# Moving two conversions of the input weights on ScalarE, and the row products ahead of the diagonal values on GpSimd, in the first loop of a fused attention and expert kernel

## The reference, cut to what matters

```python
for t in range(S):                                     # attention, B, H, S, D = 4, 8, 768, 48
    cur = np.einsum('bhd,bhe->bhde', u[None] * kt, vt)
    y[:, :, t] = np.einsum('bhd,bhde->bhe', rt, state + cur)
    state = wt[:, :, :, None] * state + np.einsum('bhd,bhe->bhde', kt, vt)
...
h = x @ w_in                                           # (3072, 384) @ (384, 2048)
g = h * np.clip(h + 3.0, 0.0, 6.0) / 6.0
x = g @ w_out
...
logits = x @ phi                                       # 32 slots, softmax over the tokens and over the slots
```

## Time and profile before

| | |
|---|---|
| median of 3 runs | 440.47 us (439.35 to 440.78) |
| the profiled execution, its own time | 439.26 us |
| its span, first to last instruction | 437.5 us |
| TensorE busy | 417.4 us, 95% |
| VectorE, ScalarE, GpSimd busy | 336.7, 155.2, 189.4 us |
| granted TensorE clock, mean | 0.972 |
| DMA traffic | 69.35 MB |

### The profile page before, as it was taken

One profiled execution on the slowest core, in us unless ns is written; L12 is line 12 of the kernel. 1 busy time (PEld: TensorE's weight loads), 2 busy tenths in 40 slices (PEclk: granted clock), 3 DMA queues, 4 the chain that ended last, 5 costly groups with the idle time before them and its releaser, 6 DMA issues.

```text
span 437.5 us, 9670 instructions
## 1 busy us (share of the span) xinstructions
PE 417.4 (95%) x3904; PEld 226.7 (52%) x3904; DVE 336.7 (77%) x529; ACT 155.2 (35%) x260; POOL 189.4 (43%) x180
## 2 busy tenths in 40 slices
PE   8998999999999999999999999989999999999973
PEld 3876555555555655555555565545554433443420
DVE  7776899998989898898889888898866676562333
ACT  2242455624333435143432433432333232231132
POOL 7524779876346556436644556544640000100000
PEclk9995999999999999999999999999999999999985
DMA  8996223338232133213330331231008961669919
GB/s 235 342 392 254 59 63 117 119 99 330 97 119 70 56 111 120 89 31 119 119 115 6 119 116 65 59 116 55 2 0 341 398 225 48 259 247 420 373 76 358
DMA packets 15245, 69.35 MB, mean 159 GB/s; under 512 B 2016, under 2 KB 2656, under 8 KB 13152
## 3 DMA queue, kind: packets, MB, share of 16 engines
q1 hardware_dynamic: 15200, 68.73, 44.4%
HBM read 64.00 MB, written 4.72 MB: 157 GB/s over the span
## 4 chain that ended last, share of the span: by engine, by line
PE 70%; issue 8%; DVE 7%; POOL 7%; DMA 4%; ACT 2%; SPq 0%; POOLq 0%; DVEq 0%
PE hid L526 12%; PE hid L528 11%; PE hid L527 11%; PE l_ps L561 5%; PE y_ps L492 4%; PE l_ps L587 4%; DMA att<-rkT_dram 4%; PE sc_ps L427 3%; PE hid L735 2%; PE inc_ps L452 2%; PE y_ps L509 2%; DVE att L797 2%; POOL w_split L1273 1%; PE sc_ps L587 1%; DVE gated L884 1%
## 5 line engine op out<-in xcount | busy, mean ns | idle before, releaser
L1151 ACT ACTIVATE relu<-hid,three 128x512 f32<-128x512 f32 x96 | 65.9, 687 | 144.0 <-PE hid L528 143.3
L526 PE MATMUL hid<-x_split,w_split 128*128 128x512 f16 x288 | 109.7, 381 | 0.0
L528 PE MATMUL hid<-x_split,w_split 128*128 128x512 f16 x288 | 109.4, 380 | 0.0
L527 PE MATMUL hid<-x_split,w_split 128*128 128x512 f16 x288 | 109.3, 380 | 0.0
L884 DVE SCALAR_TENSOR_TENSOR gated<-relu,hid 128x512 f32<-128x512 f32 x96 | 65.2, 679 | 29.4 <-ACT relu L1151 28.8
L894 DVE STREAM_TRANSPOSE ring<-gated 128x512 f32<-128x512 f32 x96 | 68.3, 711 | 3.3
L1288 POOL TENSOR_TENSOR att<-att 128x1024 f16<-128x1024 f32 x20 | 40.6, 2030 | 52.0 <-ACT att L1096 52.0
L1306 POOL TENSOR_TENSOR att<-att 112x512 f32<-112x512 f32 x19 | 22.5, 1183 | 58.7 <-DVE att L809 58.7
L526 PEld LDWEIGHTS hid<-x_split,w_split 128*128 128x128 f16 x288 | 28.2, 98 | 37.7 <-issue 10.0
L528 PEld LDWEIGHTS hid<-x_split,w_split 128*128 128x128 f16 x288 | 28.1, 98 | 34.2 <-issue 0.3
L527 PEld LDWEIGHTS hid<-x_split,w_split 128*128 128x128 f16 x288 | 28.2, 98 | 25.3 <-issue 0.6
(11 more groups left out here) (204 smaller groups left out, 756.5 us busy)
## 6 DMA issues: line engine op xcount, KB each, us to landing
att<-nat_dram SPq DMA_DIRECT2D x20, 576.0 KB, 4.1
att<-rkT_dram SPq DMA_DIRECT2D x22, 448.0 KB, 5.5
att<-w_dram SPq DMA_DIRECT2D x5, 1536.0 KB, 14.4
att<-wT_dram SPq DMA_DIRECT2D x22, 226.2 KB, 4.7
out_dram<-w_split SPq DMA_DIRECT2D x12, 384.0 KB, 3.9
stage<-w_in_dram SPq DMA_DIRECT2D x2, 1536.0 KB, 13.5
ring<-w_outT_dram SPq DMA_DIRECT2D x1, 3072.0 KB, 15.6
stage<-w_dram SPq DMA_DIRECT2D x2, 1536.0 KB, 9.2
```

Of the source, the lines that this page charges most:

```text
L526: pe.matmul(hid[s % 2][:], high, x_high, start=(q == 0), stop=False)
L527: pe.matmul(hid[s % 2][:], high, x_low, start=False, stop=False)
L528: last = pe.matmul(hid[s % 2][:], low, x_high, start=False, stop=(q == KT - 1))
L1151: nc.scalar.activation(relu_tile(s), hid[s % 2][:], ACT.Relu, bias=three[:], scale=GATE / H_SCALE)\
```

## The change

Two orders in the first loops are altered; no instruction is added or removed. On ScalarE the high parts 0 and 1 are made behind the first state of unit 1 and no longer of unit 2, and the high part 2 with its scaling behind the first state of unit 2, ahead of the keys of unit 3. On GpSimd the product of the next unit's rows stands ahead of the diagonal values of the unit and no longer behind them.

```diff
@@ -1180,11 +1180,12 @@
                     copy_diag(n + 1)
                 high_x(n)
                 first_state(n)
-                if n == 2:
+                if n == 1:
                     high_w(0)
                     high_w(1)
-            high_w(2)
-            scale_w(2)
+                if n == 2:
+                    high_w(2)
+                    scale_w(2)
             high_v(B)
             high_scores(B)
 
@@ -1338,9 +1339,9 @@
             multiply_rows(0)
             for n in range(B):
                 decay_keys(n + 1)
-                diag_values(n)
                 if n + 1 < B:
                     multiply_rows(n + 1)
+                diag_values(n)
             decay_state(B)
             decay_keys(B + 1)
             diag_products(B)
```

## The result

| | before | changed |
|---|---|---|
| median of the runs made together | 440.10 us (439.35 to 440.78, 4 runs) | 434.15 us (433.84 to 436.49, 4 runs) |
| profiled execution, its own time | 439.26 us | 434.32 us |
| its span | 437.5 us | 432.6 us |
| granted TensorE clock, mean | 0.972 | 0.994 |

The ratio of the changed kernel to the one before is 0.9899, with a 95% interval of 0.9862 to 0.9937: 4.4 us faster, between 2.8 and 6.1. The profiled executions differ by 4.9 us. The median before came out at 439.33 us in a later series of 17 runs, so the 5.95 us between the two medians above are a little too many.

The account below looks back on a forecast made before the run. TensorE, busy 95% of the span, was taken as the bound, losing time only in stops or at low clock. 2.3 + 0.1 + 3.6 + 0.65 = 6.7 us, 5.5 left after a new stop: 440.47 - 5.5 = 435.0 us, range 433.0 to 438.4.

Parts of the forecast that it names:

- The place of the cost: VectorE's 2.32 us wait at `low_w(0)` for ScalarE's high part delays `mask_first(3)`, so TensorE stops 2.77 us ahead of `attend_first(3)`.
- The mask: `mask_first(3)` on VectorE moves from 33.77 to about 31.45 us, leaving a stop of about 0.5 us on TensorE.
- GpSimd's move: `multiply_rows(1)` ahead of `diag_values(0)`: `diagonal(1)` 0.77 us sooner, `finish_y(0)` 0.8 later, worth 0.1 us at the mask.
- The clock: TensorE stays at 2.4 GHz behind the shorter stop: 3.6 us from `attend_first(3)` to `mlp(0)`, 0.65 more in `mlp(0)`.
- rival 1: The clock falls all the same, so only the wait, 2.3 + 0.1 us, is won: 438.1 us, chance 0.12.
- The collision: `low_w(1)` on VectorE, ready at 42.1 us, takes turns with GpSimd's `low_scores(4)` and ends at about 43.95.
- The stop ahead of `score(5)`: TensorE, ready at 46.1 us, waits for GpSimd's `decay_receptance(5)` until 47.35: a new stop of about 1.3 us.
- The 5.5 us stay: From `score(5)` on TensorE is full and the waits are those of before, so the 5.5 us reach the end.
- the six cases: The forecast, chance 0.5, and five rivals with chances 0.12, 0.15, 0.15, 0.04 and 0.04.
- case 3: No collision between VectorE and GpSimd: a gain of 6.5 us, 434.0 us, chance 0.15.
- Rival 4: A longer stop at `score(5)` makes the clock fall again: 1.1 us slower, 441.6 us, chance 0.04.

Follow-up runs that it names:

- e1: ScalarE's move alone, GpSimd's order kept as before, against the kernel before: 433.96 us, ratio 0.9882.
- e2: GpSimd's move alone, ScalarE's high parts made where they were, against the kernel before: 439.39 us, ratio 0.9993.
- e3: The kernel before with twelve more spare matmuls on TensorE ahead of `attend_first(3)`: 436.29 us, ratio 0.9937 to the kernel before.
- e8: e5 with `low_v(n)` on VectorE one step sooner in all later units: 454.28 us, ratio 1.0352 to the kernel before.
- e5: The changed kernel with `low_w(1)` moved on VectorE from step 0 to step 1: 433.57 us, ratio 0.987 to the kernel before.
- e9: e5 with `low_v(n)` on VectorE one step sooner in units 5 and 6 only: 433.74 us, ratio 0.9878 to the kernel before.
- e7: The kernel before with five more spare matmuls on TensorE ahead of `attend_first(3)`: 436.28 us, ratio 0.994 to the kernel before.

## Why the prediction was right, point by point

Forecast were 435.0 us and a gain of 5.5. Measured were 434.15, a gain of 4.9 by the profiled executions and of 2.8 to 6.1 by the interval; e1, the same gain with tighter runs, has 439.33 - 433.96 = 5.4. The gain is what was forecast well. That 435.0 lies only 0.85 us from 434.15 is in part luck: it starts from a median of three runs, 440.47, which 17 later runs put at 439.33, and from there the same sum gives 433.8.

- **The place of the cost.** Shown: the wait of `low_w(0)` is gone in the changed trace, and e1 and e2 give all of the gain to ScalarE's move.
- **The start.** The first loop of the changed execution began 0.35 us late, which belongs to no move. A first load landed 0.16 us later, and `scan_prefix(0)` then started 0.05 us behind the first `decay_keys` and waited for it, where before it had started 0.13 us ahead. The scan before and in the changed kernel:

```profile
5.35 1.24 DVE L809 TENSOR_TENSOR_SCAN att<-att 112x517 f32<-112x517 f32 x1
...
5.52 2.22 DVE L809 TENSOR_TENSOR_SCAN att<-att 112x517 f32<-112x517 f32 x1
```

All times forecast for the first loop have to be read with these 0.35 us.
- **The mask.** Forecast 31.45, with the late start 31.8; measured 31.81. The stop behind it: 0.5 forecast, 0.43 measured.
- **GpSimd's move.** Forecast 0.1 us. It went step by step as reckoned: `multiply_rows(1)` over 2 us long behind the scan (2.20), `diag_values(0)` pushed back, `finish_y(0)` at 14.5 and 0.35 (14.87). e2 measured no difference.
- **The clock.** `attend_first(3)` 1.96 us as said. `mlp(0)` was forecast at 37.3, with the late start 37.65, and came at 37.74. The forecast priced the clock at 3.6 + 0.65 = 4.25 us at `increment(4)`, and e3 measured 4.3 there; at the end e3 shows 3.0 us, which is rival 1's difference from the forecast (438.1 - 435.0 = 3.1). `increment(4)` itself was forecast at 42.7, with the late start 43.05, and came at 43.22.
- **The collision.** `low_w(1)` was to start at 42.1 and last nearly 2 us: 42.66 and 1.67, which is 0.75 more than 0.92. By the Trainium skill (GPSIMD Engine Reference, Key points) it had to contend with `low_scores(4)`, having two inputs in SBUF; the trace agrees, as does e8, with 2.31 us for 0.54. The stop ahead of `score(5)`: 1.3 forecast, 1.06 measured, because TensorE got there some 0.25 us later than reckoned; the start of `score(5)`, 47.35 and 0.35, was met (47.78).
- **Behind it.** "The 5.5 us stay" held for the change (384.7 and 384.8 us from `score(5)` to the end).
- **Where it was off.** Three places, none of which moved the forecast time. First, the chances given to the six cases add up to 1 and leave nothing for "what I haven't thought of". Second, case 3 gave 434.0 us for a kernel with no collision; e5 takes it away, and only about half of the 1.1 us stays, in part because `low_v(5)` meets the next product of GpSimd. Third, the prediction reckoned the clock by the length of the stop ahead of it, and length isn't all.
- **The clock and the length of a stop.** In e2, with the whole stop of 2.8 us, two of twelve executions took 436.1 and 436.5 us with a mean clock of 0.994, which are the time and the clock of the traced e3, and one of the eleven runs of the kernel before beside e8 and e9 took 436.37 us at 0.990. By that they did without the fall, though their traces weren't taken; the executions at about 439.3 us have 0.972 to 0.981. The Trainium skill (TensorE: Matmul & The Clock Gate, Part 1) says that the chip's watch over TensorE runs freely and doesn't start with the kernel, so that the moment of a change differs from run to run; that fits these, and no run here shows the watch itself. What the traces do show is the same pair of stops with and without a fall behind it. Near the end of both kernels TensorE stands for 0.78 us, works for 0.86 and stands for 1.28. Behind these stops the clock fell at about 423.5 in the kernel before, where TensorE was working again, and stayed at 1.00 to the last of its matmuls in the changed one.

In the kernel before:

```profile
422.68 0.32 PE L778 MATMUL k_ps<-w_phi,soft 96*128 96x384 f16 x1 [1.28 <-ACT w_phi L1243]
422.00:424.00 2.00, 1.16 (x6) 0.52 (x6) 1.52 (x3) 0.80 (x2) 0.00 (x0) 0.87 0.03 8
```

and in the changed one:

```profile
417.73 0.32 PE L778 MATMUL k_ps<-w_phi,soft 96*128 96x384 f16 x1 [1.28 <-ACT w_phi L1244]
418.00:420.00 2.00, 1.81 (x10) 0.59 (x7) 1.91 (x4) 1.63 (x4) 0.00 (x0) 1.00 0.18 68
```

There it cost nothing, since from `score(5)` to the end the two kernels take the same time.
- **Rival 4** (a new fall of the clock at `score(5)`) didn't come: clock 1.00 through a stop of 1.06 us in the changed kernel. Elsewhere it was 1.00 through 1.69 us in e7 and 2.10 in e8, and fell with 2.77 us (before, e2) and 2.99 (e8). A longer stop ahead of `score(5)` itself wasn't tried.

## What to carry to other kernels

When a stop of TensorE is followed by a stretch at half the clock, price the two apart: here the clock was worth 3.0 us and the wait another 2.3, and spare matmuls in the wait win the clock's share without touching the wait. Then look at what the saved time moves: work on VectorE with two inputs in SBUF and GpSimd's products take turns, so an order that brings two of them together adds to the later one what is left of the earlier. A wait that TensorE has in the middle of a chain, like the 0.79 us ahead of `diagonal(1)`, can be worth nothing (e1, e2) where another engine's queue sets the next meeting point.

## What was not expected of the hardware

- A stop of 1.69 us inside the first loop, with short matmuls on both sides, left the clock at 1.00 in the traced execution of e7 and cost nothing in four of five, and one of 2.77 us cost some 3 us in most executions but apparently not in all (e2, and the kernel before). The same two short stops near the end were followed by a fall in one trace and by none in another.
- In taking turns, the later of the two waited for the whole of the earlier: a VectorE instruction of 0.54 us that came 0.1 us after a product of 1.99 us took 2.31 us. Moving one such instruction one step sooner in every later unit made the kernel 21 us slower than e5 (e8).
